# Attention woven into the MLPs: no attention stage, transposes on VectorE and by DMA, FF blocks in pairs

## The reference

```python
kv_pool = kv.reshape(B, H // 4, 4, W // 4, 4, C).mean(axis=(2, 4))      # 768 keys a batch
k = v = kv_pool.reshape(B, -1, C) @ w_sr
s = (q @ k.transpose(0, 2, 1)) / sqrt(C)
a = exp(s - s.max(-1)); a /= a.sum(-1) + 1e-9
x = a @ v                                                               # 24,576 tokens
h = x @ w_in1;  y = (h * sigmoid(1.702 * h)) @ w_out1
h = maximum(y @ w_in2, 0);  out = (h * h) @ w_out2
```

## Time and profile before

| | us |
|---|---|
| median of 3 runs (2663.77 to 2664.49) | 2664.19 |
| span of the profiled execution | 2663.0 |
| median less span | 1.2 |
| PE busy | 2634.1 |
| ACT busy | 2117.5 |
| DVE busy | 1911.4 |
| POOL busy | 313.9 |

### The profile page before, as it was taken

One profiled execution on the slowest core, in us unless ns is written; L12 is line 12 of the kernel. 1 busy time (PEld: TensorE's weight loads), 2 busy tenths in 40 slices (PEclk: granted clock), 3 DMA queues, 4 the chain that ended last, 5 costly groups with the idle time before them and its releaser, 6 DMA issues.

```text
span 2663.0 us, 44367 instructions
## 1 busy us (share of the span) xinstructions
PE 2634.1 (99%) x12420; PEld 2218.5 (83%) x12420; DVE 1911.4 (72%) x3394; ACT 2117.5 (80%) x3998; POOL 313.9 (12%) x278
## 2 busy tenths in 40 slices
PE   6999999999999999999999999999999999999999
PEld 5999889988888888888888888888888888888887
DVE  7888888866766667676767676767666676767676
ACT  4777777778888888888888888888888888888887
POOL 3666565520000000000000000000000000000000
PEclk9999999999999999999999999999999999999999
DMA  4222211100000000000000000000000000000000
GB/s 148 83 84 83 66 59 47 47 28 13 12 12 12 12 12 12 12 12 12 12 12 12 12 12 12 16 12 12 12 12 12 12 12 12 12 12 12 12 8 12
DMA packets 40631, 67.53 MB, mean 25 GB/s; under 512 B 4512, under 2 KB 17056, under 8 KB 40608
## 3 DMA queue, kind: packets, MB, share of 16 engines
q1 hardware_dynamic: 33696, 54.67, 6.6%
q10 hardware_dynamic: 6912, 12.59, 1.2%
HBM read 42.07 MB, written 25.17 MB: 25 GB/s over the span
## 4 chain that ended last, share of the span: by engine, by line
PE 98%; DMA 1%; DVE 0%; ACT 0%; issue 0%; POOL 0%; SPq 0%; POOLq 0%; ACTq 0%
PE bank L291 29%; PE bank L293 29%; PE bank L292 29%; PE bank L347 5%; PE bank L337 5%; PE bank L353 2%; DMA kv_raw<-kv_t 1%; DVE pooled L687 0%; POOL probs_even L850 0%; DVE act_lo L764 0%; PE bank L304 0%; DVE neg_max L702 0%; ACT pt_hi L540 0%; ACT act_full L590 0%; PE bank L310 0%
## 5 line engine op out<-in xcount | busy, mean ns | idle before, releaser
L764 DVE TENSOR_TENSOR act_lo<-act_full,act_hi 128x512 fp32r<-128x512 f32 x1536 | 1056.4, 692 | 443.0 <-ACT act_full L590 416.5
L597 ACT ACTIVATE kv_raw<-bank 128x512 f32<-128x512 f32 x768 | 462.0, 602 | 214.0 <-PE bank L293 213.9
L291 PE MATMUL bank<-act_hi,w_hi 128*128 128x512 f32 x1536 | 598.0, 389 | 1.9 <-DVE in_lo L782 1.1
L293 PE MATMUL bank<-act_lo,w_hi 128*128 128x512 f32 x1536 | 597.5, 389 | 0.0
L292 PE MATMUL bank<-act_hi,w_lo 128*128 128x512 f32 x1536 | 597.5, 389 | 0.0
L291 PE MATMUL bank<-in_hi,w_hi 128*128 128x512 f32 x1504 | 585.3, 389 | 0.0
L293 PE MATMUL bank<-in_lo,w_hi 128*128 128x512 f32 x1504 | 585.1, 389 | 0.0
L292 PE MATMUL bank<-in_hi,w_lo 128*128 128x512 f32 x1504 | 585.1, 389 | 0.0
L587 ACT ACTIVATE act_hi<-bank 128x512 fp32r<-128x512 f32 x768 | 462.1, 602 | 150.7 <-PE bank L293 150.0
L775 DVE CAST act_hi<-act_full 128x512 fp32r<-128x512 f32 x768 | 327.2, 426 | 206.4 <-ACT act_full L602 199.1
L602 ACT ACTIVATE act_full<-kv_raw 128x512 f32<-128x512 f32 x768 | 474.5, 624 | 0.0
(11 more groups left out here) (62 smaller groups left out, 2256.9 us busy)
## 6 DMA issues: line engine op xcount, KB each, us to landing
kv_raw<-kv_t SPq DMA_DIRECT2D x24, 512.0 KB, 4.0
q_raw<-q_t SPq DMA_DIRECT2D x96, 128.0 KB, 2.0
x_park<-x_out ACTq DMA_DIRECT2D x48, 256.0 KB, 2.0
x_raw<-x_park SPq DMA_DIRECT2D x48, 256.0 KB, 2.6
y_t<-y_out SPq DMA_DIRECT2D x48, 256.0 KB, 2.0
w_raw<-w_all SPq DMA_DIRECT2D x16, 256.0 KB, 3.0
w_sr_sb<-w_sr SPq DMA_DIRECT2D x1, 64.0 KB, 6.0
eye_sb<-eye SPq DMA_DIRECT2D x1, 64.0 KB, 5.3
```

Source lines behind the costliest of these rows:

```text
L291: nc.tensor.matmul(out, w_parts[0], m_parts[0], start=start, stop=False)
L293: return nc.tensor.matmul(out, w_parts[0], m_parts[1], start=False, stop=stop)
L597: nc.scalar.activation(relu[:, f % H_RING, :], hidden[f % H_RING], ACT.Relu).then_inc(h_read, 1)
L764: nc.vector.tensor_tensor(act_lo[f % G_RING][:, :], act_full[:, f % H_RING, :], act_hi[f % G_RING][:, :].bitcast(F32), ALU.subtract)\
```

## The change

The attention stage is gone. A start-up part takes tiles 0 to 2 through attention (tile 2 up to its probabilities). Then `iteration(t)` runs 47 times (t from 0 to 46), each in two halves of eight pairs of FF blocks: the first half is the first MLP of tile t+1, the second half the second MLP of tile t. Between the pairs stand, on PE, the values of tile t+2 and the scores of tile t+3. The second MLP of the last tile ends the program.

The transposes leave PE. DVE transposes 32x32 blocks of the normalised probabilities (`turn`), and 16 DMAs from SBUF to SBUF, issued by SP, put the blocks where the keys are in the partitions (`move_turned`; 32 partitions x 6 x 512 bytes each), into pt_lo. ACT copies that to pt_hi and POOL subtracts in place for pt_lo. The queries are handed over in another order so that the tokens come out in order.

FF blocks go in pairs: activations, casts and subtractions are 1024 columns wide, on two PSUM banks, and the buffers hold pairs (two hidden, two of act_full, four of act_hi and act_lo). The gelu is taken once; DVE casts and subtracts for it as for the square. x stays in SBUF: ACT copies it and rounds it, POOL subtracts. There is one bank for scores, and y2 and x share a bank. All four groups are normalised on POOL. The kv of batch 0 is loaded into 12 buffers at once from two queues.

The diff, cut to its core:

```diff
-            def transpose_unit(t, c, which, projected):
-                ...
-                for j in range(SUB):
-                    last = nc.tensor.transpose(unit_bank[c % UNIT_RING][:, 128 * j:128 * j + 128],
-                                               probs[which][:, j, 128 * c:128 * c + 128], eye_sb[:, :])
+            def move_turned(a):                                   # SP
+                sp.wait_ge(turned_done, SUB * a + SUB)
+                positive(sp, x_done, a)
+                for i in range(GROUPS):
+                    src = turned[32 * i:32 * i + 32, :, :, :].rearrange("p (c g) s u -> p c g (s u)", g=GROUPS)
+                    for g in range(GROUPS):
+                        dst = pt_lo[32 * g:32 * g + 32, :, 128 * i:128 * i + 128].bitcast(F32)
+                        sp.dma_start(dst, src[:, :, g, :]).then_inc(turned_in, 16)
...
+            def up(m, f, n, source):                              # PE; n is the pair's number
+                if f % 2 == 0:
+                    positive(pe, h_read, n - 1)
+                ...
+            def down(m, f, n):
+                if f % 2 == 0:
+                    pe.wait_ge(act_split, n + 1)
+                ...
+            def pair(m, before, p, n, src, first_sum, half=None, ready=None):
+                for e in range(2):
+                    if half is not None:
+                        half(p, e)
+                    ...
+                    up(m, 2 * p + e, n, src)
+                    if p >= LAG:                                  # LAG = 3 pairs
+                        if p == LAG and e == 0:
+                            first_sum()
+                        down(m, 2 * (p - LAG) + e, n - LAG)
+                    elif before is not None:
+                        down(before, 2 * (p - LAG + PAIRS) + e, n - LAG)
+                if half is not None:
+                    half(p, 2)
...
+                def between_first(p, e):
+                    ...
+                    if values is not None and p == PAIRS - 1 and e != 1:
+                        value(t + 2, e // 2, values)
+                def between_second(p, e):
+                    if values is not None and p <= 1 and e != 1:
+                        value(t + 2, 2 + 2 * p + e // 2, values)
+                    if scores is not None and (p, e) in ((0, 0), (1, 1), (3, 0), (5, 0)):
+                        j = {0: 0, 1: 1, 3: 2, 5: 3}[p]
+                        score(t + 3, j, score_view(s_bank), SUB * (t + 3) + j)   # waits for exp j - 1
...
-                nc.scalar.activation(act_hi[f % G_RING][:, :], hidden[f % H_RING], ACT.Gelu_apprx_sigmoid)
-                ...
-                nc.scalar.activation(act_full[:, f % H_RING, :], hidden[f % H_RING], ACT.Gelu_apprx_sigmoid)\
-                    .then_inc(h_read, 1)
+            def gelu(p, n):                                       # ACT
+                act.wait_ge(h_done, n + 1)
+                positive(act, act_split, n - 1)
+                nc.scalar.activation(act_full[:, p % 2, :], h_bank[p % 2][:, :], ACT.Gelu_apprx_sigmoid)\
+                    .then_inc(h_read, 1)
...
+            def turn(a, j):                                       # DVE
+                dve.wait_ge(probs_done, SUB * a + j + 1)
+                if j == 0:
+                    positive(dve, turned_in, MOVES * a)
+                nc.vector.transpose(turned[:, :, j, :],
+                                    probs[:, j, :].rearrange("p (b u) -> p b u", u=32)).then_inc(turned_done, 1)
+            def split(p, n, ready, count):
+                dve.wait_ge(ready, count)
+                positive(dve, act_used, n - 3)
+                nc.vector.tensor_copy(act_hi[p % 4][:, :], act_full[:, p % 2, :]).then_inc(act_hi_done, 1)
+                dve.wait_ge(act_hi_done, n + 1)
+                nc.vector.tensor_tensor(act_lo[p % 4][:, :], act_full[:, p % 2, :],
+                                        act_hi[p % 4][:, :].bitcast(F32), ALU.subtract).then_inc(act_split, 1)
...
+            def iteration(t, values, scores, chunk=False, project=False):   # POOL
+                if scores is not None and not (isinstance(t, int) and t == 0):
+                    split_q_lo(t + 3)
+                if values is not None:
+                    for c in range(KC):
+                        split_pt_lo(t + 2, c)
+                for j in range(SUB):
+                    if scores is not None:
+                        normalise(t + 3, j)
+                    if j == 1 and values is not None:
+                        split_x_lo(t + 2, 0)
```

More of the change, by code:

```diff
@@ L111, in attention_mlp_mlp @@
+        w_raw = sb("w_raw", [128, KV_CHUNK])
         w_hi = sb("w_hi", [128, W_COLS], F32R)
         w_lo = sb("w_lo", [128, W_COLS], F32R)
-        x_raw = sb("x_raw", [C, TOK])
         in_hi = [sb(f"in_hi{m}", [C, TOK], F32R) for m in range(2)]
         in_lo = [sb(f"in_lo{m}", [C, TOK], F32R) for m in range(2)]
[L119 to L122, removed]
@@ L185, in loop, with first_pair, second_pair @@
[L185 to L194, removed]
+        def first_pair(t, p):
+            return 16 * t + 8 + p if not (isinstance(t, int) and t < 0) else p
+        def second_pair(t, p):
+            return 16 * t + 16 + p if not (isinstance(t, int) and t == TILES - 1) else 16 * t + 8 + p
@@ L513, in _ @@
+            iterations(pe, iteration)
+            last = TILES - 1
+            second_half(last, source(0), lambda: pe.wait_ge(y2_copied, last), before=1)
+            for p in range(PAIRS - LAG, PAIRS):
+                for e in range(2):
+                    down(1, 2 * p + e, second_pair(last, p))
         @block.scalar
         def _(act):
-            def split_q_hi(t, h):
-                act.wait_ge(q_in[h], 16 * (t + 1))
-                if not (isinstance(t, int) and t < 1):
-                    act.wait_ge(scores_done, SUB * t + 2 * h - 2)
-                nc.scalar.activation(q_hi[h][:, :], q_raw[h][:, :], ACT.Copy).then_inc(q_hi_done, 1)
@@ new lines, in _, with iteration @@
+            for c in range(KC):
+                split_pt_hi(0, c)
+            for j in range(SUB):
+                exp(2, j, early_scores[(SUB * 2 + j) % 3])
+            copy_x(0)
+            split_x_hi(0, 0, 1)
+            split_q_hi(3)
+            first_half(-1, 0, None)
+            def iteration(t, values, scores, chunk=False, project=False):
+                first_half(t, values, scores, project)
+                second_half(t, values, scores)
+            iterations(act, iteration)
@@ L834, in _ @@
-            tile_b(0, first=True)
-            loop(dve, 1, TILES - 2, tile_b)
-            tile_b(TILES - 2, last=True)
-            for f in range(FC):
-                square_split(f, LAST2 + f, FC * (TILES - 1) + f)
+                    kv_lo(0, u)
+            for j in range(SUB):
+                row_max(0, j, early_scores[j % 3])
+                if j >= 1:
+                    invert(0, j - 1)
+                if j >= 2:
+                    turn(0, j - 2)
+            invert(0, SUB - 1)
```

1037 lines of the change are left out of this document (468 added, 569 removed).

## The result

The changed kernel takes 2837.0 us (median of 4 runs, 2833.8 to 2837.9), the kernel before 2664.3: 1.0644 times as long, 95% interval 1.0631 to 1.0657. Forecast were 2572 us and "faster".

A forecast was written before the change was run, and what follows sets the result against it. The prediction took PE, busy 99% of the span, as the bound: 2496 us of work, 52 idle in the start, 4 at the end, 19 for waiting casts and 1.2 from span to median gave 2572 us; range 2540 to 2800.

The forecast's parts named there:

- PE's work: Matmuls left on PE without the transposes: 2496 us in all, 51.9 us per iteration.
- DVE beside POOL: In iterations, POOL works 17.7 us beside DVE; lengthened casts were charged 0.4 us per iteration, 19 us in all.
- So casts wait: DVE's casts and POOL's operations exclude each other; the subtraction with one input in PSUM is untouched.
- rival A: DVE's subtraction from two SBUF inputs also waits for POOL: 4.5 to 6 us per iteration, 2765 to 2835 us; chance 0.40.
- DVE has 11.5 us to spare: Argument against the subtraction waiting: spare DVE time per iteration could absorb it, leaving 1 to 2 us, 2600 to 2650.
- Behind them SP has q and y, needed many us later: In SP's queue behind the sixteen transfers, only q and y were named, neither needed soon.
- The start: Until the iteration for t = 0, at about 95 us; PE idles 52 us, against 22 before.
- the 42.7: PE's work in us before the iteration for t = 0: scores, projections, values and the first MLP blocks.
- The transfers: Sixteen per tile at 0.45 us an issue plus 2 us landing: 9.2 us, bounds 2 and 16.4.
- rival B: The transfers bind at their upper bound: 1.7 us in 45 iterations, 2649 us; chance 0.12 shared with a mild subtraction wait.
- Turn 0.95 forecast: DVE's turn of 768 columns in 32x32 blocks: between 0.62 and 1.23 us, taken as 0.95.
- the drain of which the Trainium skill speaks: About 1.38 us on each ACT table switch; by that rule gelu 0 0.4 us late, 18 us over the iterations.

The follow-up runs named there:

- micro: Not the kernel: VectorE operations alone, then beside GpSimd subtracting 512 columns, then transfers; beside it the cast goes from 0.77 to 1.69 us, the two-SBUF-input subtraction 1.25 to 2.22.
- kv_ahead: Changed kernel with the kv chunk load issued on SyncE ahead of the sixteen transfers of its iteration: 2767.0 us, 1.038 of the kernel before.
- q_ahead: Changed kernel with the start's loads of q tiles 2 and 3 issued ahead of the transfers of tiles 0 and 1: 2831.1 us, 1.0621 of the kernel before.
- w_on_vector: Changed kernel with VectorE instead of GpSimd casting and subtracting the first eight weight chunks in the start: 2832.0 us, 1.0624 of the kernel before.
- best: Changed kernel with kv load, score 0 maximum and q loads ahead, tile 0's last turn and tile 1's casts earlier, eight weight chunks on VectorE: 2617.6 us.
- moves_four: Changed kernel with four transfers of 32 partitions x 12 KB for the sixteen, transposition left incomplete: 2777.7 us, 1.0422 of the kernel before.

## Why the prediction was wrong

- *PE's work: right.* 51.9 us per iteration forecast, 52.1 measured where PE never waits. The transposes' 125 us did go.
- *DVE beside POOL: the step that failed.* "So casts wait" left the subtraction out, since the earlier trace rows show it only with one input in PSUM, where it is indeed immune. From two SBUF inputs it excludes POOL as the cast does (micro). The steady wait, 3.5 us over PE's work instead of the 0.4 charged, is some 47 x 3.1 = 146 us. That was rival A, with the right place (the maximum behind the last gelu split) and first size (1.9 us forecast at score 1, 1.66 measured). Its later waits were too high: 55.6 us steady is 3.7 over 51.9, below its 4.5 to 6. That 2837 lies just beyond its 2835 is so only because the next two items fill the gap. "DVE has 11.5 us to spare", which spoke against A, was no answer to it: DVE was busy 48.1 us per steady iteration where 40.4 were forecast, 4 under PE's 52.1, and even a true sum says nothing of the queue ahead of one maximum.
- *"Behind them SP has q and y, needed many us later": false.* In twelve iterations the kv chunk stands there too, and DVE wanted it 2.7 us before it was even issued. kv_ahead gives 70 us back; my own sum named the queue and did not list what is on it. No term and no rival had it.
- *The start: 95 forecast, 126.3 measured* (127.8 less 1.5). The transfers of tile 0 began at 45.7 and landed at 57.7, not 48, because the last turn stood behind the first maximum of tile 1, and the q loads for tiles 2 and 3 stood behind transfers. The first up came at 75.7 instead of 64.5, its gelu only at 85.8, and from that up to t = 0 it took 51 us where I had 30. Of the 31.3 us more, 12 are idle time (64.0 instead of 52), for which POOL's load and the order were both at fault (q_ahead, w_on_vector, best). The other 20 are busy time (63.8 where the 42.7 and the 1.5 were forecast), and that term was priced at the pitches of the full clock. In the start the mean granted clock is 0.83: behind its pauses PE's matmuls come 0.43 us apart instead of 0.23, which adds some 15 us over 85 of them (the first up, below). POOL's own prices, which the forecast took from shapes half as wide, were too high rather than too low (pt_lo 1.48, measured 1.26). Even best starts t = 0 at 109.4, 13 us behind the forecast.

```profile
75.73 0.76 PE L260 MATMUL h_bank<-in_hi,w_hi 128*128 128x512 f32 x1 [4.61 <-issue]
76.29 0.63 PE L261 MATMUL h_bank<-in_hi,w_lo 128*128 128x512 f32 x1
76.72 0.63 PE L262 MATMUL h_bank<-in_lo,w_hi 128*128 128x512 f32 x1
```

- *The transfers: size off, consequence small.* 0.65 us between issues instead of the 0.45 of the earlier trace rows, so 12 us instead of 9.2, within the bounds. 2.4 us less of it gave 0.35 us per steady iteration (moves_four); rival B did not bind.
- *Turn 0.95 forecast, 0.97 measured; cast 0.70, 0.69 alone; subtraction 1.23, 1.23 alone: right.* The table load is 1.28 us as in the earlier trace rows, and the exponential starts 0.02 after it, so without the drain of which the Trainium skill speaks (ScalarE: Activation LUTs, What ACT_TABLE_LOAD costs): right.
- The chance of 0.40 for "slower" was on the right mechanism. The prediction named a rule for A and had no row against it, so the forecast should have leaned on A.
- Open: t = 0 takes 60 us in every version, with POOL splitting eight weight chunks beside it; that was not taken apart.

## What to carry to other kernels

Before work is moved onto GpSimd, list each VectorE operation that may run beside it by where its inputs lie: here a cast and a subtraction from two SBUF inputs each grew by 0.9 us per encounter, one with an input in PSUM, a 32x32 transposition and a maximum from PSUM by nothing. Then ask of each queue, SyncE's too, what is the first thing behind the lengthened or added block that another engine waits for, iteration kind by iteration kind; busy shares don't tell. And when a mend gives little, try it with the others before dropping it: 70, 104 and 6 us alone were 206 together.

## What the runs showed of the hardware that I had not expected

- An issue of 32 x 6 blocks of 512 bytes takes SP 0.61 us, with 0.65 between issues; four issues of the same 1.5 MB in rows of 12 KB take 4.5 us, the last two being held back, and land 9.5 us after the first. Sixteen small ones land 12.1 us after it: a quarter of the issues saved only 2.6 us.
- A pause of 7 us costs PE more than itself: some seven matmuls after it ran at the lower clock, 1.5 us on top.
- Work done by DVE itself (0.61 us pitch per pt_lo) is cheaper for DVE than the same work done beside it by POOL (0.9 us per encounter): its busy time fell from 48.1 to 46.5 us per steady iteration though it did six operations more.
